# Two spare columns in front of the later weights

## The chip, the cores and the metric

One NeuronCore of a Trainium2 chip runs the whole program. The metric is the time of one execution on the device in microseconds (us); the figures below are of three executions and of one more that was profiled.

## The reference

The inputs are q, k, v of shape (4 batches, 8 heads, 576 positions, 64) and the matrices of two feed-forward layers. All is float32.

```python
scores = q @ k.T / 8 + slope[head] * -(i - j)      # kept where 0 <= i - j < 128
attn   = softmax(scores) @ v                       # -> x: 2304 tokens x 512
h = x @ w_in;  x2 = (h * sigmoid(1.702 * h)) @ w_out                 # 512 -> 2048 -> 512
h = x2 @ w_in2
g = where(h >= 1, h, where(h <= -1, 0, (h + 1)**2 / 4));  out = g @ w_out2
```

The first layer uses `moe_w_in`, `moe_w_out`, the second `moe2_w_in`, `moe2_w_out`.

## The kernel before, in words

Attention comes first and takes the first 138 us of the profiled span. The rest is matrix products of the two layers. They are written as Strassen products: of each 2x2 block product seven products remain (P1 to P7), and both factors of each are sums or differences of quadrants. Each factor is split into a high part, rounded to the type fp32r, and a low part (what the rounding left). A product is then three matmuls for each 128-deep slice: high x high, high x low, low x high.

The layers run in four phases `u` (two for each layer, each half of the 2048 hidden features). A phase has an up part (three chunks of 768 tokens, two "duos" for each chunk) and a down part (three chunks, one duo each). A duo is the fourteen calls of `multiply` (L1057 and after) for seven products and two positions. In the up parts, and in the down parts of phases 0 and 1, a piece of weights is the stationary operand (128 columns are loaded into the array) and 384 columns of activations move through it. In the down parts of phases 2 and 3 (`swapped`) the activations are stationary and 256 columns of weights move.

There are four tiles on SBUF that the change or its prediction speaks of. They are listed with their starts, in bytes of each partition, in the program as built:

- `w_first`, 1216: weight sets of slots 0, 1 and 2. One set is seven operands, each of 2 x 256 columns (high and low), 14336 bytes.
- `arena`, 44288: the split activations, all parts a multiple of 512 bytes apart.
- `w_rest`, 130368: weight sets of slots 3, 4 and 5. Its size is 43008 bytes.
- behind it `g` at 173376, `ust` at 197952 and `raw_rest` at 210240; before it `d1s` at 124224.

Weight set `w` lies in slot `w % 6` (`w_place`), so each phase uses both tiles. The three tiles of matmul operands begin at multiples of 64 bytes. `w_first` and `w_rest` begin 64 bytes behind a multiple of 128, `arena` at a multiple of 128. They differ further: modulo 256, `w_first` is at 192, `w_rest` at 64 and `arena` at 0. Two pads of 64 bytes (`before_w_first`, `before_arena`) stand in front of the first two.

ScalarE rounds the high part of a weight set (L1309, L1312) and VectorE takes the low part (L1682, L1687), both straight into `w_place(w)`. Six sets that don't fit are made early and kept in device memory; SyncE loads them back into their place with seven transfers each (`load_stock`, L628). SyncE issues all loads and stores of the layers, in an order written out by hand; each waits on a semaphore for the buffer that it fills. `g` holds the hidden activations on their way to device memory, `raw_rest` half of the activations on their way back, `ust` the outputs.

The order of TensorE's instructions is fixed by hand as well. The matmul of the layers is one line:

```python
last = nc.tensor.matmul(to, stationary, moving, start=start and n == 0, stop=n == len(steps) - 1,   # L1075
```

Of the kernel before, what the change touches and what calls it, by code (L numbers as in the profile page):

```python
# [21 lines left out]
F32R = mybir.dt.float32r  # L22
# [3 lines left out]
P = 128  # L26
# [71 lines left out]
OPS = 7  # L98
# [14 lines left out]
def build(nc, qkT, v_main, v_tail, w_pairs, bias_table, identity, out):  # L113
# [3 lines left out]
    def sb(name, shape, dt, into=ctx):  # L117
        return into.enter_context(nc.sbuf_tensor(name, shape, dt))
# [39 lines left out]
    attn_ctx.close()  # L158

    d1s = sb("d1s", [P, 2, 2 * HALF], F32)  # L160
    w_rest = sb("w_rest", [P, 3, OPS, 2, 2 * P], F32R)
    g = sb("g", [P, 2, 4, 2 * HALF], F32)
    ust = sb("ust", [P, 4, 2 * HALF], F32)
    raw_rest = sb("raw_rest", [P, 3, 4 * HALF], F32)
# [1892 lines left out]
```

## Time and profile before

| | |
|---|---|
| median of 3 executions | 852.87 us (852.66 to 853.97) |
| profiled execution, its own time | 852.58 us |
| its span, first to last instruction | 850.8 us |
| TensorE matmul (PE), busy | 843.7 us |
| VectorE (DVE), busy | 711.4 us |
| ScalarE (ACT), busy | 538.5 us |
| GpSimd (POOL), busy | 116.4 us |
| granted TensorE clock, mean | 0.999 |

Matmuls overlap each other in the records: one of 384 columns lasts 336 ns, and the next one starts about 174 ns after it. So the time that a matmul costs is the distance between starts, and that can be read from a timeline that merges equal neighbours: the start of one row is taken from the start of the next and divided by the first row's count.

### The profile page before, as it was taken

Reading aid. Unit: us, or ns where it says so; the run is one execution under the profiler, and the core shown is the slowest. Engines: PE = TensorE matmul, PEld = TensorE weight load, DVE = VectorE, ACT = ScalarE, POOL = GpSimd, SP = SyncE. Lnnn points to the kernel's source line nnn. Section 1 sums busy time; section 2 is a strip of 40 time slices with the busy share of each in tenths; the row PEclk is TensorE's granted clock in tenths of the full one; section 3 lists DMA queues with packets and bytes.
Section 4 is the critical chain, followed back from the end, with each engine's and each line's share of the span. In section 5 each row is a group of like instructions: output and inputs, shape, how many; then the busy total and the mean of one; then the engine's idle time right before and its main releaser. Section 6 shows DMA issues by size and latency. Waiting matters only on the chain.

```text
span 850.8 us, 15510 instructions
## 1 busy us (share of the span) xinstructions
PE 843.7 (99%) x5744; PEld 839.7 (99%) x5744; DVE 711.4 (84%) x982; ACT 538.5 (63%) x791; POOL 116.4 (14%) x82
## 2 busy tenths in 40 slices
PE   8999999999999999999999999999999999999998
PEld 8999999999999999999999999999999999999998
DVE  7888898786988966778998987989989788889794
ACT  7778787767775546768644556767555567665441
POOL 3788988000000000000000000000000000000000
PEclk9999999999999999999999999999999999999999
DMA  8888661667676347687764772587647643888822
GB/s 203 226 213 217 191 180 67 268 253 277 250 253 226 133 150 272 250 303 240 260 246 184 287 242 105 210 282 260 235 152 262 231 154 128 291 294 304 310 83 75
DMA packets 63257, 186.45 MB, mean 219 GB/s; under 512 B 7504, under 2 KB 14352, under 8 KB 59344
## 3 DMA queue, kind: packets, MB, share of 16 engines
q1 hardware_dynamic: 62896, 185.30, 63.3%
q8 instruction: 47, 0.77, 0.3%
q14 instruction: 26, 0.21, 0.1%
q10 hardware_dynamic: 288, 0.16, 0.1%
HBM read 113.09 MB, written 72.35 MB: 218 GB/s over the span
## 4 chain that ended last, share of the span: by engine, by line
PE 92%; DVE 5%; POOL 1%; issue 1%; ACT 0%; DVEq 0%; POOLq 0%
PE ps L1075 79%; PE ps L1043 4%; PE ps L1009 3%; PE ps L1022 3%; DVE arena L1755 1%; PE ps L972 1%; POOL qk_hi L895 1%; PE ps L1037 1%; POOL k_lo L892 1%; PE ps L1052 1%; DVE probs L1645 1%; DVE qk_hi L1613 0%; DVE raw_first L1714 0%; DVE g L1787 0%; DVE raw_first L1709 0%
## 5 line engine op out<-in xcount | busy, mean ns | idle before, releaser
L1075 PE MATMUL ps<-arena,w_first 128*128 128x384 f32 x1764 | 328.6, 336 | 0.0
L1075 PEld LDWEIGHTS ps<-arena,w_first 128*128 128x128 f32 x1764 | 307.2, 188 | 0.9 <-DVE arena L1755 0.3
L1075 PE MATMUL ps<-arena,w_rest 128*128 128x384 f32 x1260 | 241.4, 336 | 0.0
L1075 PEld LDWEIGHTS ps<-arena,w_rest 128*128 128x128 f32 x1260 | 221.8, 188 | 0.6 <-issue 0.3
L1755 DVE TENSOR_TENSOR arena<-raw_first,arena 128x768 fp32r<-128x768 f32 (+1 forms) x114 | 148.8, 1318 | 75.8 <-ACT arena L1333 75.8
L1333 ACT ACTIVATE arena<-raw_first 128x768 fp32r<-128x768 f32 (+1 forms) x120 | 131.9, 1118 | 46.1 <-DVE raw_first L1714 39.7
L1075 PE MATMUL ps<-w_rest,arena 128*128 128x256 f32 x945 | 131.9, 280 | 0.6 <-DVE g L1858 0.6
L1075 PEld LDWEIGHTS ps<-w_rest,arena 128*128 128x128 f32 x945 | 120.0, 188 | 0.8 <-issue 0.8
L1075 PE MATMUL ps<-w_first,arena 128*128 128x256 f32 x567 | 85.8, 278 | 0.0
L1755 DVE TENSOR_TENSOR arena<-raw_rest,arena 128x1536 fp32r<-128x1536 f32 (+1 forms) x48 | 71.3, 1485 | 7.8 <-ACT arena L1333 7.7
L1333 ACT ACTIVATE arena<-raw_rest 128x1536 fp32r<-128x1536 f32 (+1 forms) x48 | 60.9, 1268 | 22.4 <-PE ps L1075 20.3
L1075 PEld LDWEIGHTS ps<-w_first,arena 128*128 128x128 f32 x567 | 74.8, 188 | 0.0
L1379 ACT ACTIVATE d1s<-ps 128x384 f32<-128x384 f32 (+2 forms) x72 | 35.3, 491 | 39.8 <-PE ps L1075 39.7
L1247 ACT ACTIVATE probs<-probs,neg_max 128x256 f32<-128x256 f32 (+1 forms) x128 | 54.1, 472 | 6.9 <-DVE neg_max L1645 6.9
L1043 PE MATMUL ps<-v_sb,probs_t 128*128 128x65 f32 x448 | 57.0, 268 | 0.5 <-DVE heads_out L1658 0.5
L1043 PEld LDWEIGHTS ps<-v_sb,probs_t 128*128 128x128 f32 x448 | 55.3, 191 | 0.9 <-issue 0.8
L1645 DVE CUSTOM_DVE_ANT_0 probs<-ps,bias_sb 128x256 f32<-128x256 f32 (+1 forms) x128 | 44.6, 387 | 13.3 <-PE ps L1009 8.7
L1370 ACT ACTIVATE ps<-ps 128x384 f32<-128x384 f32 (+2 forms) x72 | 34.2, 476 | 28.8 <-PE ps L1075 27.7
L1677 DVE TENSOR_TENSOR wst<-wst 128x256 f32<-128x256 f32 (+1 forms) x90 | 48.5, 539 | 2.8
L1287 ACT ACTIVATE probs_t<-ps 128x512 f32<-128x512 f32 x64 | 37.8, 590 | 18.4 <-PE ps L1022 18.1
L1009 PE MATMUL ps<-qk_hi 128*128 128x256 f32 x158 | 47.7, 324 | 1.0 <-POOL qk_hi L895 0.4
L895 POOL TENSOR_TENSOR qk_hi<-qk_raw,qk_hi 64x576 fp32r<-64x576 f32 x28 | 45.1, 1612 | 2.2
(125 smaller groups left out, 971.4 us busy)
## 6 DMA issues: line engine op xcount, KB each, us to landing
gd<-g SPq DMA_DIRECT2D x24, 1536.0 KB, 6.1
raw_rest<-gd SPq DMA_DIRECT2D x32, 768.0 KB, 5.2
wst<-w_pairs SPq DMA_DIRECT2D x32, 512.0 KB, 5.7
raw_first<-gd SPq DMA_DIRECT2D x16, 768.0 KB, 5.8
yd<-ust SPq DMA_DIRECT2D x6, 1536.0 KB, 6.3
qk_raw<-qkT SPq DMA_DIRECT2D x30, 288.0 KB, 3.8
wd<-ust SPq DMA_DIRECT2D x4, 1536.0 KB, 8.7
raw_first<-yd SPq DMA_DIRECT2D x4, 1536.0 KB, 6.7
```

Source lines behind the costliest of these rows:

```text
L895: nc.gpsimd.tensor_tensor(all_queries(qk_hi, head, LOWER), all_queries(qk_raw, head, UPPER), f32(all_queries(qk_hi, head, UPPER)), ALU.sub ...
L1009: last = nc.tensor.matmul(place, queries, k[:, key0:key0 + BAND], start=n_pass == 0 and (d > 0 or i == 0), stop=n_pass == 1 and (d > 0 or ...
L1043: last = nc.tensor.matmul(o_slot(2 * blk + e), probs_t[:, gi % 2, col:col + P], v_sb[:, h + e, max(blk - 1, 0) + piece], start=piece == 0, ...
L1075: last = nc.tensor.matmul(to, stationary, moving, start=start and n == 0, stop=n == len(steps) - 1, skip_group_check=True)
L1247: last = nc.scalar.activation(at, at, ACT.Exp, bias=neg_max[:, col:col + 1], scale=-1.0)
L1287: nc.scalar.activation(probs_t[:, gi % 2], pt_bank[gi % 2], ACT.Copy).then_inc(pt_copied[gi % 2], 1)
L1333: nc.scalar.activation(operand(k, i)[:, 0], source(k, i), ACT.Copy).then_inc(hi_made, 1)
L1370: nc.scalar.activation(b_bank(D, pos), a_bank(D, pos), ACT.Copy).then_inc(seeded_b, 1)
L1379: nc.scalar.activation(d1(D, pos), d_bank(D, pos), ACT.Copy).then_inc(d_copied, 1)
L1645: last = nc.vector.tensor_tensor_reduce(out=to[:, 0:width], in0=bank[:, i * BAND:i * BAND + width], in1=bias_sb[:, h + e, BAND - width:BAN ...
L1677: nc.vector.tensor_tensor(to, a, b, ALU.subtract).then_inc(w_added, 1)
L1755: nc.vector.tensor_tensor(at[:, 1], source(k, i), f32(at[:, 0]), ALU.subtract).then_inc(lo_made, 1)
```

## The change

The tile `w_rest` gets two float32 columns more in front, and the weight sets begin behind them. All that reads or writes `w_rest` uses the new view. Slots 3, 4 and 5 so lie 8 bytes further on: their start goes from 130368 to 130376. `w_first`, `arena` and all that lies before `w_rest` keep their places. Tiles begin at multiples of 32 bytes, so `g`, `ust` and `raw_rest` behind it go 32 bytes on (173408, 197984, 210272). No instruction is added or taken away, and no size, order or wait changes.

```diff
     d1s = sb("d1s", [P, 2, 2 * HALF], F32)
-    w_rest = sb("w_rest", [P, 3, OPS, 2, 2 * P], F32R)
+    w_rest_line = sb("w_rest", [P, 2 + 3 * OPS * 4 * P], F32R)
+    w_rest = w_rest_line[:, 2:].rearrange("p (s o h n) -> p s o h n", s=3, o=OPS, h=2)
     g = sb("g", [P, 2, 4, 2 * HALF], F32)
```

## Rows read from the trace of the kernel before

**Rows 1.** The page: span, busy time, slices with TensorE's granted clock.
```profile
span 850.8 us, 15510 instructions
PE 843.7 (99%) x5744; PEld 839.7 (99%) x5744; DVE 711.4 (84%) x982; ACT 538.5 (63%) x791; POOL 116.4 (14%) x82
...
PEclk9999999999999999999999999999999999999999
```

**Rows 2.** The page: chain that ended last, by engine.
```profile
PE 92%; DVE 5%; POOL 1%; issue 1%; ACT 0%; DVEq 0%; POOLq 0%
```

**Rows 3.** Who waited for whom, TensorE alone (total us, times, longest).
```profile
PE ps L972 <- DVE arena L1578: 1.4, 1, 1.4
PE ps L1075 <- DVE g L1858: 0.6, 1, 0.6
```

**Rows 4.** Groups by line and shape: L1075's matmuls with each weight tile.
```profile
L1075 PE MATMUL ps<-arena,w_first 128*128 128x384 f32 x1764 | 328.6, 336 | 0.0
...
L1075 PE MATMUL ps<-arena,w_rest 128*128 128x384 f32 x1260 | 241.4, 336 | 0.0
...
L1075 PE MATMUL ps<-w_rest,arena 128*128 128x256 f32 x945 | 131.9, 280 | 0.6 <-DVE g L1858 0.6
...
L1075 PE MATMUL ps<-w_first,arena 128*128 128x256 f32 x567 | 85.8, 278 | 0.0
```

**Rows 5.** Timeline of TensorE, up part of phase 2: start, length, count.
```profile
509.06 14.72 PE L1075 MATMUL ps<-arena,w_first 128*128 128x384 f32 x84
523.62 14.84 PE L1075 MATMUL ps<-arena,w_rest 128*128 128x384 f32 x84
538.30 14.73 PE L1075 MATMUL ps<-arena,w_first 128*128 128x384 f32 x84
552.87 14.84 PE L1075 MATMUL ps<-arena,w_rest 128*128 128x384 f32 x84
567.54 14.73 PE L1075 MATMUL ps<-arena,w_first 128*128 128x384 f32 x84
```

**Rows 6.** Timeline of TensorE, down parts of phases 2 and 3.
```profile
620.63 1.22 PE L1075 MATMUL ps<-w_rest,arena 128*128 128x256 f32 x9
621.69 0.51 PE L1075 MATMUL ps<-w_first,arena 128*128 128x256 f32 x3
...
820.32 0.85 PE L1075 MATMUL ps<-w_first,arena 128*128 128x256 f32 x6
821.00 0.87 PE L1075 MATMUL ps<-w_rest,arena 128*128 128x256 f32 x6
821.71 0.85 PE L1075 MATMUL ps<-w_first,arena 128*128 128x256 f32 x6
```

**Rows 7.** Busy time of TensorE in the whole down parts of phases 2 and 3.
```profile
582.10:671.20 89.10, 89.10 (x759) 1.00 0.60 211
758.90:847.50 88.60, 87.99 (x757) 1.00 0.56 198
```

**Rows 8.** Timeline around 523.5 us: the weight loads (PEld) and their matmuls (PE).
```profile
523.45 2.11 PEld L1075 LDWEIGHTS ps<-arena,w_rest 128*128 128x128 f32 x12
523.62 2.08 PE L1075 MATMUL ps<-arena,w_rest 128*128 128x384 f32 x11
```

**Rows 9.** Groups by shape: the writers of `w_rest` (ScalarE and VectorE).
```profile
L1687 DVE TENSOR_TENSOR w_rest<-wst,w_rest 128x1536 fp32r<-128x1536 f32 x12 | 21.0, 1752 | 2.1 <-ACT w_rest L1312 2.0
...
L1312 ACT ACTIVATE w_rest<-wst 128x1536 fp32r<-128x1536 f32 x12 | 17.9, 1488 | 2.5 <-DVE wst L1677 2.5
```

**Rows 10.** Who waited for whom, all engines: the longest.
```profile
DVE arena L1755 <- ACT arena L1333: 83.5, 46, 4.7
```

**Rows 11.** DMA issues: size of each, median us from issue to landing.
```profile
gd<-g SPq DMA_DIRECT2D x24, 1536.0 KB, 6.1
raw_rest<-gd SPq DMA_DIRECT2D x32, 768.0 KB, 5.2
...
w_rest<-wd SPq DMA_DIRECT2D x21, 256.0 KB, 4.6
```

**Rows 12.** Timeline of TensorE in attention: groups of 65 columns of v_sb.
```profile
60.62 1.00 PE L1043 MATMUL ps<-v_sb,probs_t 128*128 128x65 f32 x8
...
68.67 1.00 PE L1043 MATMUL ps<-v_sb,probs_t 128*128 128x65 f32 x8
...
76.74 1.00 PE L1043 MATMUL ps<-v_sb,probs_t 128*128 128x65 f32 x8
```

## The prediction

> **What bounds the kernel now.** I read the page first: TensorE is busy for 843.7 of 850.8 us, and its clock is granted in full in all 40 slices [rows 1]. The chain that ended last lies on TensorE for 92% [rows 2], and TensorE's own waits come to a few parts of a microsecond once the layers run (0.6 us is the only one at L1075) [rows 3]. So it is TensorE's stream of matmuls that takes the time, and an edit moves the end only by a change in the distance between two starts, or by a wait that does not exist today.
>
> Next, what that distance is. The groups by shape give the counts: 3024 matmuls move 384 columns, 1764 of them with stationary weights from `w_first` and 1260 from `w_rest`; 1512 move 256 columns of weights, 567 from `w_first` and 945 from `w_rest` [rows 4]. Their mean lengths overlap, so they are no price. The timeline gives one. In the up part of phase 2 the weights come from one tile for a whole duo of 84 matmuls [rows 5]: from `w_rest` (538.30 - 523.62)/84 = 174.8 ns and (567.54 - 552.87)/84 = 174.6 ns, from `w_first` (523.62 - 509.06)/84 = 173.3 ns and (552.87 - 538.30)/84 = 173.5 ns. At the granted 2.4 GHz, one column a cycle, 384 columns are 160.0 ns. So each matmul carries 14.7 ns on top with `w_rest`, 13.4 ns with `w_first`. For 256 moving columns (106.7 ns) the rows give (621.69 - 620.63)/9 = 117.8 ns from `w_rest`, and (821.00 - 820.32)/6 = 113.3 ns from `w_first`; the six after them from `w_rest` give 118.3 ns [rows 6]. That is 11.1 ns on top against 6.6 ns.
>
> These rows are the heart of the case. Shapes, types, engines and neighbours are the same; what differs is the tile from which the weights are read. `w_first` and `w_rest` start at the same place modulo 128 bytes and at different ones modulo 256. So the place of a weight tile already shows in the distance between starts, by 1.3 ns in one use and 4.5 ns in the other. The change moves just this for 2205 of 4536 matmuls, by an amount (8 bytes) for which the trace has no fp32r row: all fp32r operands begin at multiples of 64 bytes now.
>
> **The change part by part.**
>
> *Weights from `w_rest`, stationary (1260 matmuls).* Ends first. Below: all of the 14.7 ns goes, 1260 x 14.7 = 18.5 us less. Above: it doubles, 18.5 us more. The nearest row with another place is `w_first`, 1.3 ns less: 1260 x 1.3 = 1.6 us less. I take this.
>
> *Weights from `w_rest`, moving (945 matmuls).* Below: the 11.1 ns goes, 10.5 us less; above: doubles, 10.5 us more. Nearest row, `w_first`: 4.5 ns less, 945 x 4.5 = 4.3 us less. As a check on whole stretches: the down part of phase 2 has 9 of every 12 matmuls from `w_rest` and takes 89.10/756 = 117.9 ns each; phase 3 has 6 of 12 and is busy for 87.99/756 = 116.4 ns each [rows 7]. 1.5 ns for a quarter of the matmuls is 6.0 ns for one, so 4.5 is not high. I take 4.3 us.
>
> Why the same sign as `w_first` at all? A weight load starts 0.17 us ahead of its own matmul [rows 8], which is the distance between two starts: so it runs with the matmul before it, and both read SBUF. The tiles now start at equal places within 64 bytes, so the two reads keep step; the 14.7 and 11.1 ns are there although nothing is waited for. A start half of 16 bytes off puts the two out of step for `w_rest`. That is an argument for less, not a price; the price is what the other tile shows.
>
> *Writers of `w_rest`.* ScalarE and VectorE write each set once: 12 of 1488 ns and 12 of 1752 ns for the large parts [rows 9]. Should they be slower by a tenth, it is 12 x 0.15 + 12 x 0.18 = 3.9 us of engine time in all, spread over 700 us. VectorE waits 83.5 us for ScalarE at L1755 alone [rows 10], and TensorE waits for neither: it is hidden, 0. Uncovered, one set would be late by 0.3 us.
>
> *Transfers.* The 21 stock loads into `w_rest` land in 4.6 us, `raw_rest` in 5.2 us, a store of `g` takes 6.1 us [rows 11]. These tiles move by 8 or 32 bytes. A store or load of 768 KB that costs a tenth more would land 0.5 us later. What hides it is the same: TensorE has no wait on a load in the layers [rows 3]. I take 0; the bound is the one place where TensorE does wait, 0.6 us before L1858's result, which could come to 1.8 us: 1.2 us more. No gain is possible here, since there is no wait to lose.
>
> Sum: 1.6 + 4.3 = 5.9 us less. The profiled execution took 852.58 us, 1.8 us around its span of 850.8, and is 0.3 us under the median of 852.87. So 852.58 - 5.9 = 846.7 for it, and 846.9 to 847.0 for the median. I predict 847.0 us.
>
> A rule that speaks against this: the Trainium skill (page "SBUF — State Buffer", section "SBUF: two separate sides") says that SBUF is read in lines of 16 bytes, that a line should be hit at least twice, and that each step to a new line costs. By that rule an operand of 128 columns at an offset of 8 bytes touches 33 lines instead of 32 and one of 256 columns 65 instead of 64, with two hits in the first and last line, so a small loss and never a gain, at most the slower time that the first rival below works out from rows. The trace shows nothing on it for fp32r; it is carried as the first rival.
>
> **The rivals.**
>
> *The read is cut in one more piece (slower).* An operand that begins off the border of whatever piece is fetched at once needs one piece more at its end. The price by rows: with 16-byte pieces a stationary operand has 32, and if the 14.7 ns are their cost, one more is 0.5 ns; a moving one of 64 pieces in 106.7 ns pays 1.7 ns. 1260 x 0.5 + 945 x 1.7 = 2.2 us more: 855.1. With 64-byte pieces it is 14.7/8 = 1.8 ns and 106.7/16 = 6.7 ns: 2.3 + 6.3 = 8.6 us more: 861.5. I put the case at 857. It decides from the point where an extra piece isn't taken up by the 11 to 15 ns that are there anyway. For it: the distance between starts is set by reads, not by waits. Against: attention reads v_sb at pieces of 260 bytes, so groups of eight begin at offsets of 0, 4, 8 and 12 bytes within 16, and all last 1.00 us [rows 12]; but a 65-column matmul takes some 110 ns there, with time to spare for one more read.
>
> *Out of step altogether (much faster).* If the extra time is two reads that meet again at each step, half or all of it goes for `w_rest`: half is 0.5 x (18.5 + 10.5) = 14.5 us, 838.4; all is 29 us, 823.9. For it: extras of 11 to 15 ns on a matmul that waits for nothing. Against: `w_first` and `w_rest` differ by more than nothing at equal places within 128 bytes, so keeping step within 16 bytes is not the whole story.
>
> *Nothing.* If only the place at the scale of 128 or 256 bytes counts, 8 bytes change nothing and the time stays within 0.2%: 852.9. v_sb's equal groups speak for it.
>
> **How the numbers follow.** About 0.2%, 1.7 us, is what a measurement of this kernel can tell from no change. Forecast (a gain of 2 to 10 us): 0.33. Much faster: 0.17. Nothing: 0.20. One more piece: 0.30. So faster 0.50, same 0.20, slower 0.30. The forecast's own range is 843 to 851. For 8 in 10 the range goes on to 838 (half of the extra gone, some 0.1 left below it) and 858 (the middle of the slower case, some 0.1 above). The doubling at 29 us more is left out.
>
> **What would show it.** In the up part of phase 2 the two rows of 84 with `w_rest` shorten to 14.56 us from start to start (or 14.8 and more under the first rival, 14.1 and less under the second), while the three with `w_first` stay at 14.56 or so. In the down parts, nine matmuls from `w_rest` take 1.02 instead of 1.06 us. TensorE's waits stay as they are, and ScalarE's 1488 and VectorE's 1752 ns for `w_rest` stay within a few ns. The prediction is wrong if the `w_rest` rows lengthen, if the `w_first` rows move as much as they do, or if the time goes into a new wait of TensorE on a load.

## The result and the profile after

| | before | after |
|---|---|---|
| median | 852.86 us (6 runs, 852.48 to 853.97) | 856.35 us (6 runs, 855.24 to 856.65) |
| ratio, with its 95% interval | | 1.0034 [1.0024, 1.0043] |
| span of the profiled execution | 850.8 us | 854.7 us |

The change makes the kernel 3.5 us slower. I had forecast 847.0 us, 5.9 us faster. The time lies within the range, near the 857 us of the first rival, on the other side of no change from the forecast.

The page of the kernel after is first. With the two new lines of code, the matmul of the layers is L1076 now. These rows answer to [rows 1].

```profile
span 854.7 us, 15510 instructions
PE 847.5 (99%) x5744; PEld 843.5 (99%) x5744; DVE 711.6 (83%) x982; ACT 538.9 (63%) x791; POOL 116.4 (14%) x82
...
PEclk9999999999999999999999999999999999999999
```

TensorE's busy time grew from 843.7 to 847.5 us, by as much as the span (3.8 and 3.9 us); the other engines stand within 0.4 us of before and the clock is granted in full again. Who waited for whom, TensorE alone (total us, times, longest), answers to [rows 3]:

```profile
PE ps L1076 <- DVE g L1859: 0.5, 1, 0.5
```

The other wait of [rows 3], 1.4 us at the start of the program, is as before, and there is no new one. So the time went where the prediction looked for it, into the distance between two starts, with the other sign. The timeline of the up part of phase 2 (start, length, count), which answers to [rows 5]:

```profile
509.26 14.72 PE L1076 MATMUL ps<-arena,w_first 128*128 128x384 f32 x84
523.82 14.91 PE L1076 MATMUL ps<-arena,w_rest 128*128 128x384 f32 x84
538.57 14.72 PE L1076 MATMUL ps<-arena,w_first 128*128 128x384 f32 x84
```

From start to start the rows with `w_rest` take 14.75 us (before 14.68), 175.6 ns a matmul, and those with `w_first` 14.56 us, 173.3 ns, as before. The two down parts in which weights move, phase 2 (answers to the first rows of [rows 6]) and phase 3, where TensorE waits once for VectorE:

```profile
620.39 1.26 PE L1076 MATMUL ps<-w_rest,arena 128*128 128x256 f32 x9
621.48 0.52 PE L1076 MATMUL ps<-w_first,arena 128*128 128x256 f32 x3
621.83 1.26 PE L1076 MATMUL ps<-w_rest,arena 128*128 128x256 f32 x9
...
788.58 0.84 PE L1076 MATMUL ps<-w_first,arena 128*128 128x256 f32 x6
789.26 0.88 PE L1076 MATMUL ps<-w_rest,arena 128*128 128x256 f32 x6
...
792.68 0.96 PE L1076 MATMUL ps<-w_rest,arena 128*128 128x256 f32 x6 [0.46 <-DVE g L1859]
793.47 0.87 PE L1076 MATMUL ps<-w_first,arena 128*128 128x256 f32 x6
794.18 0.89 PE L1076 MATMUL ps<-w_rest,arena 128*128 128x256 f32 x6
```

Nine matmuls from `w_rest` take 621.48 - 620.39 = 1.09 us, where it was 1.06; twelve take 1.44 instead of 1.41. In phase 3 the six from `w_first` take 789.26 - 788.58 = 0.68 us, as in the row of before, until TensorE's wait for VectorE. Behind it they take 794.18 - 793.47 = 0.71 us, although that tile was not moved. Over all of phase 3 a matmul costs 116.8 ns ahead of that wait and 119.6 behind it; in the kernel before it is 116.1 and 116.3 on the two sides of the same wait. So nearly all of phase 3's loss lies behind one stall. Length and TensorE's busy time of these two down parts, with the same columns as [rows 7]:

```profile
582.40:673.60 91.20, 91.20 (x759) 1.00 0.59 205
761.20:851.30 90.10, 89.64 (x757) 1.00 0.56 196
```

The two stretches are 91.20 + 90.10 = 181.3 us long where they were 89.10 + 88.60 = 177.7 us: 3.6 us, nearly the whole loss. Starts of all 4536 matmuls, taken part by part, say the same. The parts whose moving operand is `arena` changed by between -0.24 and +0.20 us each, with a sum of nothing: `w_rest` behind `w_rest` grew from 174.6 to 175.5 ns, while the step from a `w_first` matmul to a `w_rest` one shrank from 177.4 to 171.7 ns. With 256 columns, `w_rest` behind `w_rest` went from 118.1 to 121.1 ns, and `w_first` behind `w_first` from 115.2 to 117.1.

### The profile page after: what moved, and what is told of

Its sections match the earlier page's. It is cut to its first block, busy times and chain, and to the rows that moved or that the text cites. A ratio compares the mean times of both kernels' runs of the same rounds, so it can differ in the third digit from the quotient of the medians.

```text
span 854.7 us, 15510 instructions
## 1 busy us (share of the span) xinstructions
PE 847.5 (99%) x5744; PEld 843.5 (99%) x5744; DVE 711.6 (83%) x982; ACT 538.9 (63%) x791; POOL 116.4 (14%) x82
## 4 chain that ended last, share of the span: by engine, by line
PE 90%; DVE 5%; POOL 1%; issue 1%; SPq 1%; DMA 0%; ACT 0%; DVEq 0%; POOLq 0%
PE ps L1076 79%; PE ps L1044 4%; PE ps L1010 3%; PE ps L1023 2%; DVE arena L1756 1%; POOL qk_hi L896 1%; PE ps L1038 1%; POOL k_lo L893 1%; PE ps L1053 1%; DVE probs L1646 1%; DMA v_sb<-v_tail 0%; DVE qk_hi L1614 0%; DVE raw_first L1715 0%; DVE g L1788 0%; DVE raw_first L1710 0%
## 5 line engine op out<-in xcount | busy, mean ns | idle before, releaser
L1076 PE MATMUL ps<-arena,w_first 128*128 128x384 f32 x1764 | 327.5, 336 | 0.0
L1076 PEld LDWEIGHTS ps<-arena,w_first 128*128 128x128 f32 x1764 | 307.0, 188 | 0.8 <-issue 0.2
L1076 PE MATMUL ps<-arena,w_rest 128*128 128x384 f32 x1260 | 242.5, 338 | 0.0
L1076 PEld LDWEIGHTS ps<-arena,w_rest 128*128 128x128 f32 x1260 | 222.2, 188 | 0.6 <-issue 0.3
L1076 PE MATMUL ps<-w_rest,arena 128*128 128x256 f32 x945 | 135.0, 284 | 0.5 <-DVE g L1859 0.5
L1076 PEld LDWEIGHTS ps<-w_rest,arena 128*128 128x128 f32 x945 | 122.6, 191 | 0.6 <-issue 0.6
L1076 PE MATMUL ps<-w_first,arena 128*128 128x256 f32 x567 | 86.9, 280 | 0.0
L1076 PEld LDWEIGHTS ps<-w_first,arena 128*128 128x128 f32 x567 | 76.1, 190 | 0.0
```

## The experiments

The quoted texts call the theories by letters, and say in words what each expects. Theory A is the prediction's first rival, a fixed price for a start off the border of a piece. B says that only the place of one operand against the other counts. C says that the price is not in TensorE's reads at all, but comes from what shares the memory with them. E came up during the work: successive reads lock into one of a few distances, and which one depends on the places modulo 256 bytes and on how the stream was entered. Places below are given modulo 256: before, `w_rest` lay at 64, `w_first` at 192, `arena` at 0; after, `w_rest` lies at 72.

### Matmuls alone

The kernel leaves out all of the reference's work: it multiplies zeros, in sections of 48 matmuls in a row, and only the place of the operands differs between sections (`m` for the moving one, `s` for the stationary one). The other engines are idle from 27.6 us on; one store of the outputs is issued then and moves bytes until about 40 us, beside the first two sections of 256 columns.

```diff
+        for n in range(48):
+            to, by, at, start, stop = step(n, 256, 0, 0)     # columns, m / 4, s / 4
+            nc.tensor.matmul(to, by, at, start=start, stop=stop)
```

> Only matmuls of zeros in fp32r and a store of zeros: attention and both layers are left out. Sections of 48 matmuls each, with the order of reads of the layers, the moving operand at 0, 4, 8, 16, 32, 64, 72, 128, 192 or 200 bytes within 256 and the stationary one at 0 to 200; 256 or 384 moving columns. Theory A (a moving operand that begins inside a piece of 16 bytes costs one read more): with 256 moving columns the distance between starts is about 117 ns at 0, 16, 32, 64, 128 and 192 bytes and 2 to 5 ns more at 4, 8, 72 and 200; a stationary operand at 8 bytes costs under 1 ns. Theory B (place matters only relative to the other operand): moving and stationary both at 8 bytes is as quick as both at 0, and one at 8 is slower whichever it is. Theory C (nothing in TensorE alone; the loss comes from the other engines and transfers): all sections with the same count of columns are equal within 0.5 ns.

The timeline of this kernel has one row for each section. First stand 256 columns, with s = 0 and m = 16 (L165), 64 (L171), 72 (L174), 128 (L177), 192 (L180) and 200 (L183), then 384 columns, with m = 0 and s = 64 (L213), 72 (L216), 192 (L219) and 200 (L222):

```profile
45.73 5.60 PE L165 MATMUL ps<-moved,held 128*128 128x256 f32 x48
...
56.77 5.82 PE L171 MATMUL ps<-moved,held 128*128 128x256 f32 x48
62.42 5.94 PE L174 MATMUL ps<-moved,held 128*128 128x256 f32 x48
68.20 5.92 PE L177 MATMUL ps<-moved,held 128*128 128x256 f32 x48
73.96 5.62 PE L180 MATMUL ps<-moved,held 128*128 128x256 f32 x48
79.42 5.92 PE L183 MATMUL ps<-moved,held 128*128 128x256 f32 x48
...
141.43 8.48 PE L213 MATMUL ps<-moved,held 128*128 128x384 f32 x48
149.75 8.59 PE L216 MATMUL ps<-moved,held 128*128 128x384 f32 x48
158.18 8.48 PE L219 MATMUL ps<-moved,held 128*128 128x384 f32 x48
166.50 8.59 PE L222 MATMUL ps<-moved,held 128*128 128x384 f32 x48
```

The section with m = 64 (L171) begins at 56.77 and the next at 62.42: 5.65 us, 117.7 ns a matmul; 72 takes 5.78 us, 120.4 ns. Within the sections, where the stream is steady, the distances are 117.8 and 120.0 to 120.2 ns, and at 192 they settle at 113.3. These are close to the kernel's own: 117.8 for `w_rest` and 113.3 for `w_first` before [rows 6], 121.1 for `w_rest` behind `w_rest` after. With 384 columns s = 64 and 192 give 173.3, 72 and 200 give 175.5 to 175.6 ns. So the price arises in a stream of matmuls by itself, which ends C. It isn't one more piece either: moving at 8 settles at the 117.8 ns of 64, and moving at 128 (68.20 to 73.96 us), on every border of 16 to 128 bytes, takes 120.0 ns, more than at 16 (113.3). Moving at 0 has 120.0 ns as well, beside the store and, in the finer map below, also when the store is over. The slowest is moving at 4, 123.3 ns.

### The tiles behind `w_rest` alone

```diff
-    w_rest = sb("w_rest", [P, 3, OPS, 2, 2 * P], F32R)
+    w_rest_line = sb("w_rest", [P, 0 + 3 * OPS * 4 * P + 2], F32R)
+    w_rest = w_rest_line[:, 0:0 + 3 * OPS * 4 * P].rearrange(...)
```

> The two columns stand behind the weights instead of in front: w_rest keeps its start, g, ust and raw_rest still move by 32 bytes. Theory A (the loss is the place of the weights): ratio 1.000 within 0.001, the whole down parts of phases 2 and 3 take 89.1 and 88.6 us as before. Theory D (the loss comes from the three tiles behind, by their DMAs): 1.003 to 1.004 as with the change.

853.41 against 853.32 us, ratio 1.0002 [0.9993, 1.0011]. That `g`, `ust` and `raw_rest` move by 32 bytes costs nothing within that interval; the 8 bytes of the weights are the loss. The larger shifts of these tiles in the kernels below were not tested by themselves.

### 16 bytes and 128 bytes

The first kernel has 4 spare columns in front (`w_rest` at 80), the second 32 (at 192, which is `w_first`'s place).

```diff
+    w_rest_line = sb("w_rest", [P, 4 + 3 * OPS * 4 * P], F32R)      # the second: 32
+    w_rest = w_rest_line[:, 4:4 + 3 * OPS * 4 * P].rearrange(...)
```

> Four columns in front instead of two: the later weights lie 16 bytes on, g, ust and raw_rest 32 bytes as with the change. If the piece is 16 bytes the loss is gone: 852.9 us, ratio 1.000 within 0.001. If the piece is 32 or 64 bytes it stays: 856 us or so, and down parts of 91 and 90 us.

854.97 us, ratio 1.0020 [1.0012, 1.0029]. The 16-byte piece predicts no loss at a start on its border, and half of the loss is still there. That form of A falls. A piece of 32 or 64 bytes, which should have kept all of it (856 us), is not what came either.

> 32 columns in front: the later weights lie 128 bytes on, at 192 modulo 256 as w_first does. If w_first's shorter distance (113.3 against 117.8 ns with 256 moving columns) is due to its place modulo 256, all rows with w_rest come down to w_first's: 5 to 6 us less, 847, ratio 0.993. If it is due to which matmuls follow each other, or to a higher part of the address, nothing changes: ratio 1.000 within 0.001.

850.15 us, ratio 0.9970 [0.9959, 0.9981]: faster than before, and 3 us short of the forecast. All `w_rest` matmuls of 384 columns came to 173.3 ns, `w_first`'s distance, as the forecast had priced them. The moving ones came to 117.8 ns, not to 113.3, through phase 2 and the first third of phase 3. The timeline of the down part of phase 3:

```profile
787.29 0.87 PE L1076 MATMUL ps<-w_rest,arena 128*128 128x256 f32 x6
788.00 0.87 PE L1076 MATMUL ps<-w_first,arena 128*128 128x256 f32 x6
789.07 0.94 PE L1076 MATMUL ps<-w_rest,arena 128*128 128x256 f32 x6 [0.20 <-DVE g L1859]
789.84 0.84 PE L1076 MATMUL ps<-w_first,arena 128*128 128x256 f32 x6
790.52 0.84 PE L1076 MATMUL ps<-w_rest,arena 128*128 128x256 f32 x6
```

Up to 788.00 each six take 0.71 us (0.707 over the whole stretch), 117.8 ns a matmul, with either tile. Then TensorE waits once for VectorE, and from 789.84 on each six take 0.68 us, 113.3 ns, to the end of the part. Between them lies the short stall; tiles, places and order are the same. The load of the DMA engines does not tell the two apart: their share is 0.66 from 775 to 785 us, at 117.8 ns, and 0.79 from 800 to 810 us, at 113.3 ns. This row made theory E, and the wait for VectorE in the kernel after had already shown the same kind of step.

### How the stream is entered

Matmuls of zeros again, all of the reference left out: sections of 36 alike, each behind one matmul of 128 to 158 columns, which shifts the moment of entry.

```diff
+        nc.tensor.matmul(ps[:, 7, 0:130], held[:, 0:P], moved[:, 0:130], start=True, stop=True)
+        for n in range(36):
+            to, by, at, start, stop = step(n, 256, 48, 0)    # moving at 192
+            nc.tensor.matmul(to, by, at, start=start, stop=stop)
```

> Again only matmuls of zeros; attention and both layers are left out. 64 sections of 36 matmuls, each behind one matmul of another width (128 to 158 columns), which moves the section's start in time against the stream before it. Sixteen sections with 256 moving columns at 192 bytes (widths in steps of 2), eight each at 64, 72 and 200 bytes, and eight each with 384 columns and the stationary operand at 192, 64 and 72 bytes (widths in steps of 4). Theory A (the place alone sets the distance between starts): each place has one distance, whatever the width ahead: 113.3 ns at 192, 117.8 at 64, 120.2 at 72, 120.0 at 200; 173.3 ns for 384 columns at 64 and 192, 175.6 at 72. Theory E (the two reads of SBUF lock into one of several alignments in time, and the place only says which are open): sections of one place fall into two or more distances, 113.3 and 117.7 ns among them at 192, by the width ahead.

Timeline: sections with the moving operand at 192, behind 128, 130 and 132 columns.

```profile
29.28 4.29 PE L157 MATMUL ps<-moved,held 128*128 128x256 f32 x36
33.41 0.22 PE L158 MATMUL ps<-moved,held 128*128 128x130 f32 x1
33.47 4.45 PE L161 MATMUL ps<-moved,held 128*128 128x256 f32 x36
37.76 0.22 PE L162 MATMUL ps<-moved,held 128*128 128x132 f32 x1
37.82 4.31 PE L165 MATMUL ps<-moved,held 128*128 128x256 f32 x36
```

4.13, 4.29 and 4.15 us to the next matmul: one and the same section runs at 113.3 or at 117.8 ns, by the two or four columns in front of it. The distance is the steady one at the end of a section. Of 16 such sections 6 ran at 113.3 and 10 at 117.8, with nothing between. At 64 all ran at 117.8, at 72 all but one at 120.0 to 120.3 (the one at 122.2), at 200 all at 120.0. With 384 columns the stationary operand at 192 always gave 173.3, at 72 always 175.6, and at 64 it gave 173.3, 174.7 or 176.7. The kernel before has 174.6 to 174.8 for `w_rest` at 64 [rows 5]. E holds against A here: one place (192) has two distances, and 72 never had the short one in eight entries.

### `w_first` by 8 bytes, all three tiles by 8 bytes

```diff
-    w_first = sb("w_first", [P, 3, OPS, 2, 2 * P], F32R)
-    sb("before_arena", [P, 16], F32)
+    w_first_line = sb("w_first", [P, 2 + 3 * OPS * 4 * P], F32R)
+    w_first = w_first_line[:, 2:].rearrange(...)
+    sb("before_arena", [P, 8], F32)
```

> Only w_first goes on by 8 bytes (to 200 modulo 256); w_rest, arena and all else stay. Theory E by the bare sections (113.3 to 120.0 ns when moving, 173.3 to 175.5 when stationary, for a start at 200 instead of 192): 567 x up to 6.7 = 3.8 and 1764 x 2.2 = 3.9 us more, 857 to 860.5 us, with more of it in the up parts than the change had. Theory A (one 16-byte piece more, 3 ns a moving matmul, nothing on the stationary side): 567 x 3 = 1.7 us more, 854.5.

858.48 us, ratio 1.0064 [1.0051, 1.0077]. In the up part of phase 2 the `w_first` rows of 84, not the `w_rest` ones, are the long ones now, as the timeline shows:

```profile
511.30 14.91 PE L1076 MATMUL ps<-arena,w_first 128*128 128x384 f32 x84
526.04 14.84 PE L1076 MATMUL ps<-arena,w_rest 128*128 128x384 f32 x84
540.71 14.90 PE L1076 MATMUL ps<-arena,w_first 128*128 128x384 f32 x84
```

14.74 us, 175.5 ns each, where they had 14.56, and the `w_rest` row has 14.67 as before. Moving `w_first` by 8 bytes costs 5.1 us where its 2331 matmuls are 106% of `w_rest`'s 2205 and so would cost 3.7 by a fixed price. `w_first` leaves a better place (173.3 and 113.3 ns) than `w_rest` did (174.6 and 117.8) and arrives at as bad a one (175.5 and 120 in the bare sections), as E has it: it had forecast 857 to 860.5 us, A 854.5.

The other kernel moves `w_rest` and `arena` by 8 bytes as well, so that every operand lies as before against the others.

> w_first, arena and w_rest all go on by 8 bytes, so the distances between the operands are those of before. Theory B (only the place of one operand against the other counts): ratio 1.000, 852.9 us. Theory E by the bare sections with both at 8 bytes (120.15 ns at 256 columns against 119.9 with both at 0; 173.4 against 173.3): within 0.3% of before. Theory A (an operand that begins inside a piece costs one read more, wherever the other is): all 4536 moving operands pay, some 3 ns each, 13 us more, 866.

865.83 us, ratio 1.0150 [1.0136, 1.0164]. B falls: with equal relative places it should have been no change. The time is A's number (866), but not A's mechanism, a fixed 3 ns for every moving operand. In phase 2 the rows of 84 with `w_first` take (529.55 - 514.63)/84 = 177.6 ns, 4.2 more than before, those with `w_rest` (544.31 - 529.55)/84 = 175.7 ns, 1.0 more; the moving weights cost 3.3 ns more in phase 2 and 4.3 in phase 3. E's bare sections for both operands at 8 had promised ±0.3% and that missed too. They held no pair of one operand at 8 and the other at 72 or 200, which is what this kernel has.

### A finer map, and a place chosen by it

A map in steps of 16 bytes (zeros, the reference's work left out), each place entered three times: 256 columns with the moving operand, 384 with the stationary one at each of 16 places.

```diff
+        for n in range(36):
+            to, by, at, start, stop = step(n, 256, 28, 0)    # moving at 112
```

> Matmuls of zeros alone, attention and both layers left out; sections of 36 behind one of 128, 134, 136, 140 or 142 columns. 256 moving columns at every multiple of 16 bytes within 256, and 384 with the stationary operand at every multiple of 16. By theory E each place has its own set of distances; 120.0 ns for 256 at 0, 113.3 or 117.8 at 192, 117.8 at 64; 173.3 for 384 at 192, up to 176.7 at 64. If the sets go with the place modulo 64 or 128, the rows repeat with that step; if modulo 256, they do not. Open is whether any place has a distance under 113.3 and 173.3 ns in all its sections.

Timeline: moving at 112 (L241, L245), then at 192 (L301, L305), with the odd matmuls between them.

```profile
120.04 4.33 PE L241 MATMUL ps<-moved,held 128*128 128x256 f32 x36
124.21 0.22 PE L242 MATMUL ps<-moved,held 128*128 128x134 f32 x1
124.27 4.35 PE L245 MATMUL ps<-moved,held 128*128 128x256 f32 x36
128.46 0.23 PE L246 MATMUL ps<-moved,held 128*128 128x142 f32 x1
...
185.41 4.33 PE L301 MATMUL ps<-moved,held 128*128 128x256 f32 x36
189.58 0.23 PE L302 MATMUL ps<-moved,held 128*128 128x134 f32 x1
189.65 4.46 PE L305 MATMUL ps<-moved,held 128*128 128x256 f32 x36
193.94 0.23 PE L306 MATMUL ps<-moved,held 128*128 128x142 f32 x1
```

At 112 the two sections shown take 4.17 and 4.19 us to the next matmul, and the third as much (113.3 ns within each); at 192 the first takes 4.17, the second 4.29 (117.8). Of the 16 places only 112 had 113.3 each time; 16 had 116.7 to 118.6 (113.3 in the first kernel of zeros), 0 and 96 had 120.0. Equal places modulo 64 or 128 don't have equal distances. With 384 columns, stationary at 112 gave 173.3 three times. Nothing lay under 113.3 or 173.3.

So both weight tiles went to 112, `arena` stays at 0:

```diff
-    sb("before_w_first", [P, 16], F32)
+    w_first_line = sb("w_first", [P, 60 + 3 * OPS * 4 * P], F32R)
+    w_first = w_first_line[:, 60:].rearrange(...)
-    sb("before_arena", [P, 16], F32)
+    sb("before_arena", [P, 32], F32)
...
+    w_rest_line = sb("w_rest", [P, 12 + 3 * OPS * 4 * P], F32R)
+    w_rest = w_rest_line[:, 12:].rearrange(...)
```

> Both weight tiles begin at 112 modulo 256, the arena at 0 as before; the one place where the bare sections gave 113.3 and 173.3 ns whatever stood ahead of them. Theory E: all 1512 matmuls with 256 moving columns at 113.3 ns (now 117.8 and 116.2 on average in phases 2 and 3) and all 3024 with 384 at 173.3: 5.6 + 1.6 us less, 846 us, ratio 0.991 to 0.993. If the place of the operands were not the cause, 852.9.

849.04 us, ratio 0.9958 [0.9945, 0.9970]: the fastest median of all, 7.3 us under the kernel after and 3.8 us under the one before by their own medians. But 3 us of what I expected are missing, and its five runs spread from 848.79 to 851.46, while the kernel with 16 bytes has all eleven within 0.74 us and the one before spreads over 1.5. TensorE's busy time in the down parts of phases 2 and 3, columns as in [rows 7]; then a stretch of the timeline of an up part of phase 1, then of phase 2:

```profile
585.70:671.40 85.70, 85.70 (x758) 1.00 0.62 218
758.90:846.10 87.20, 85.86 (x757) 1.00 0.58 202
```

```profile
329.20 2.29 PE L1076 MATMUL ps<-arena,w_rest 128*128 128x384 f32 x12
331.33 1.21 PE L1076 MATMUL ps<-arena,w_first 128*128 128x384 f32 x6
332.38 1.20 PE L1076 MATMUL ps<-arena,w_rest 128*128 128x384 f32 x6
333.42 1.20 PE L1076 MATMUL ps<-arena,w_first 128*128 128x384 f32 x6
...
511.00 15.10 PE L1076 MATMUL ps<-arena,w_first 128*128 128x384 f32 x84
525.93 15.10 PE L1076 MATMUL ps<-arena,w_rest 128*128 128x384 f32 x84
```

The moving weights are where the map put them: 85.70 us for 756 matmuls, 113.4 ns, and 3.4 us less than the 89.10 of before. Phase 3 is busy 85.86 of 87.20 us; TensorE now comes early and waits 1.3 us for VectorE's result (L1859). The 384-column matmuls have two distances in one execution: (331.33 - 329.20)/12 = 177.5 ns up to 331.33, 1.04/6 = 173.3 from 332.38 on, with no stall between them (the order of the tiles changes there from twelve in a row to six), and (525.93 - 511.00)/84 = 177.7 again in phase 2, where the two tiles took 173.3 and 174.8 before [rows 5]. The map's three sections at 112 had not shown the long one. The profiled execution is the slowest of the five, 851.46.

### The same 8 bytes from other places

If A holds, 8 bytes cost the same from anywhere. Two pairs put it to the test: 34 spare columns (at 200) against the 32 above (at 192), and 50 (at 8) against 48 (at 0).

```diff
+    w_rest_line = sb("w_rest", [P, 34 + 3 * OPS * 4 * P], F32R)     # the others: 48, 50
+    w_rest = w_rest_line[:, 34:].rearrange(...)
```

> The 8 bytes again, but on top of cols32: the later weights at 200 modulo 256 instead of 192. Theory E by the bare sections: 1260 x 2.2 = 2.8 us for the stationary ones (173.3 to 175.5 ns) and 945 x 3.3 = 3.1 us for the moving ones (116.7 to 120.0), 856 us, 5 to 6 more than cols32's 850.15. Theory A (a fixed 3 ns for a moving operand off the 16-byte border, nothing for the stationary one): 2.8 us more, 853.

> The later weights at 0 modulo 256, where moving weights had 120.0 ns in every bare section and stationary ones 173.3. Theory E: 945 x 2 = 1.9 us more in the down parts of phases 2 and 3, 1260 x 1.3 = 1.6 less elsewhere: 853, ratio within 0.002 of 1.

> The later weights at 8 modulo 256. Theory E by the one bare section at that place (118.0 ns moving instead of 120.0 at 0, 173.3 stationary at both): 8 bytes are no loss here but a gain of 1.9 us against cols48. Theory A (any operand that begins inside a piece of 16 bytes pays): 2 to 3 us more than cols48.

| `w_rest` from, to | spare columns | 8 bytes cost |
|---|---|---|
| 64 to 72 | 0, 2 | +3.5 us (852.86 to 856.35) |
| 192 to 200 | 32, 34 | +5.4 us (850.15 to 855.52) |
| 0 to 8 | 48, 50 | -1.6 us (854.63 to 853.06) |

The ratios to the kernel before are 1.0025 [1.0016, 1.0035] for 34 columns, 1.0015 [1.0006, 1.0024] for 48, and 0.9999 [0.9990, 1.0008] for 50. Those intervals hold the spread of the kernel before. Set directly side by side, all eleven executions at 8 (852.75 to 853.44 us) are faster than all eleven at 0 (854.40 to 855.01), so the gain is clear of the spread. A fixed price for one more piece is not there. E forecast sign and size of the two new pairs (5 to 6 us more, 1.9 us less; the first pair was known), but for the last one by the wrong term: I expected the gain in the moving use (120 to 118 ns). It came in the stationary one (175.7 to 173.4), while the moving one went the other way (117.6 to 120.0). So its number there was luck. In the kernel with 48 columns alone both terms had come with the other sign than forecast (moving 117.6 for 118.1 ns, stationary 175.7 for 174.6). The bare sections at 0 and 8 don't carry over to the kernel, as those at 64, 72, 112, 192 and 200 roughly do for the moving use. In the kernel with 50 columns the `w_rest` rows of phase 2 are as short as `w_first`'s, on a start that is 8 bytes off every border of 16:

```profile
522.76 14.72 PE L1076 MATMUL ps<-arena,w_rest 128*128 128x384 f32 x84
537.33 14.72 PE L1076 MATMUL ps<-arena,w_first 128*128 128x384 f32 x84
```

## Why the prediction was wrong

*What bounds the kernel: right.* TensorE's stream of matmuls takes the time, and the change acts through the distance between starts alone. Busy time and span grew by 3.8 and 3.9 us.

*Weights from `w_rest`, moving: this step failed.* I took `w_first`'s row as the nearest, "the price is what the other tile shows", and so 4.5 ns less for each of 945 matmuls. The row was near in all but the one thing that decides, the place: `w_first` is 128 bytes away modulo 256, the change goes 8. The bare matmuls give 117.8 ns at 64, 120.2 at 72 and 113.3 at 192, and the kernel after has 121.1. Measured, the term is 945 x 3.0 = 2.8 us more where I had 4.3 us less. The step also let `w_rest`'s matmuls pay alone; its neighbours from `w_first` paid some 567 x 1.9 = 1.1 us more, most of it behind the stall of phase 3. The sum is 3.9 us, against 3.6 in the windows, in which TensorE's wait is 0.15 us shorter. And it took one price for one place, where the same tiles had two prices on the two sides of a stall.

*Weights from `w_rest`, stationary: sign wrong, nearly no weight.* 1.3 ns less was forecast, 0.9 ns more came for `w_rest` behind `w_rest` (175.5 for 174.6), and the steps between the tiles gave it back: 0.0 us in all. Why the two cancel stays open.

*The check on whole stretches* (6.0 ns for one, so 4.5 is not high) was good arithmetic on the wrong question: it priced the difference between the two tiles, and says nothing of a place between or beside them.

*The argument of keeping step*, "A start half of 16 bytes off puts the two out of step", falls as a reason for less. 8 bytes made it slower from 64 and from 192, and faster from 0.

*Writers, transfers, tiles behind: right at 0.* With the tiles behind shifted and the weights not, ratio and windows are those of before. VectorE's large writes went from 1752 to 1754 ns, ScalarE's from 1488 to 1495 [rows 9], and TensorE's wait is 0.5 for 0.6 us.

*The first rival* had the size (857 for 856.35), not the mechanism. The piece of 16 bytes falls with the kernel at 80, the fixed price with the pair at 0 and 8, where it would be a loss. The Trainium skill's rule behind it (page "SBUF — State Buffer", section "SBUF: two separate sides": lines of 16 bytes, a penalty for each step to a new one) leaves starts at multiples of 16 alike; the runs have 113.3 to 120.0 ns among such starts, so the measurement decides that the rule does not order these cases. *The second rival* (838) fell: the least distances seen anywhere are 113.3 and 173.3 ns, so 6.7 and 13.3 ns on top of the columns remain at every place tried, where all or half should have gone from 11.1 and 14.7 ns. *Nothing* was wrong for the moving use; for the stationary use its zero came by steps that cancel.

Shown: the distance depends on the places of both operands (the map, and all three tiles at 8) and on how the stream was entered (the stalls, the odd matmuls). Not settled: how much of the 3.5 us belongs to the place and how much to the state that the stall of phase 3 leaves behind; another entry could cost up to 1.6 us less (492 x (119.6 - 116.3) ns, an estimate from the profiled execution). Not settled either: that 256 bytes is the whole period. The map's rows do not repeat in steps of 64 or 128, and the kernel's moving tiles at 64, 72, 112 and 192 modulo 256 agree with it; those at 0 and 8 don't. Only argued, from [rows 8]: that what locks are the reads of the moving and of the next stationary operand. Moving and stationary use of `w_rest` were not set apart by giving each its own place: it would have needed other synchronization, and was not tried.

## What to carry to other kernels

Before a tile of matmul operands is moved, measure the distance between starts for the new place with matmuls alone, with both operands where the kernel has them and with several ways to enter the stream; a row of another tile that lies elsewhere is no price, not even for the sign. An offset is not good or bad by its alignment: the same 8 bytes cost 5.4 us, cost 3.5 us and gained 1.6 us. And a place with two distances makes a kernel's time depend on its stalls. How much a change elsewhere moves it by that was not measured; the spread of the kernel with both tiles at 112, 2.7 us or 0.3%, may be of this kind.

## What the runs showed of the hardware that was not expected

- At the full granted clock, bare matmuls of 256 fp32r columns with a new stationary operand for each came every 113.3 to 123.3 ns by the place of their operands, those of 384 every 173.3 to 177.2 ns. At the granted 2.4 GHz 113.33 is 272 cycles and 173.33 is 416; 16 and 32 cycles on top of one cycle a column are the least seen.
- Two streams of the same instructions and places ran 4% apart (113.3 and 117.8 ns), each steady for its whole section, and in the kernel for 265 matmuls on one side of a stall and 492 on the other. Two or four columns more in one matmul ahead chose between them.
- The distance can also change with no stall that the profile shows: 177.5 to 173.3 ns at 332 us in the kernel with both tiles at 112, where the order of the tiles changes.
- A tile that was not moved can pay for one that was: `w_first`'s six moving matmuls took 0.68 us ahead of one stall and 0.71 us behind it, with `w_rest` 8 bytes further on.
